# Score products of a two-stage attention and MoE kernel: the keys' low part in half-row products, two heads in turn

## The reference

```python
scores = scale * np.matmul(q, k.transpose(0, 1, 3, 2))
...
scores = scores + bias.transpose(2, 0, 1)[None, :, :, :]
scores = scores - np.max(scores, axis=-1, keepdims=True)
attn = np.exp(scores)
attn = attn / (np.sum(attn, axis=-1, keepdims=True) + 1e-09)
return np.matmul(attn, v)
...
for e in range(E):
    h = np.maximum(x @ w1[e], 0.0)
    ye = h @ w2[e]
    out += P[:, e:e + 1] * ye
```

## Time and profile before

| | us |
|---|---|
| median of 3 runs | 1846.01 (1845.95 to 1847.39) |
| the profiled execution | 1847.22 |
| its span, first to last instruction | 1845.4 |
| TensorE busy in the span | 1829.7 |
| attention, first score product to first expert product | about 61 to 344 |

### The profile page before, as it was taken

One profiled execution on the slowest core, in us unless ns is written; L12 is line 12 of the kernel. 1 busy time (PEld: TensorE's weight loads), 2 busy tenths in 40 slices (PEclk: granted clock), 3 DMA queues, 4 the chain that ended last, 5 costly groups with the idle time before them and its releaser, 6 DMA issues.

```text
span 1845.4 us, 27892 instructions
## 1 busy us (share of the span) xinstructions
PE 1829.7 (99%) x10223; PEld 1592.1 (86%) x10223; DVE 1053.4 (57%) x1784; ACT 824.8 (45%) x1416; POOL 1028.3 (56%) x720
## 2 busy tenths in 40 slices
PE   8999999999999999999999999999999999999999
PEld 4677777788999999999999999999999999999998
DVE  8877777777554555456645554555455445544553
ACT  8777777533433333334333333333333333333331
POOL 0223326577666666666776666666666666666661
PEclk9999999999999999999999999999999999999999
DMA  7763562021112211212121211111121111112110
GB/s 241 226 155 92 128 152 68 23 79 59 69 69 69 69 69 69 69 69 103 69 69 69 69 69 69 69 69 69 69 103 69 69 69 69 69 69 69 69 46 35
DMA packets 44127, 152.47 MB, mean 83 GB/s; under 512 B 9584, under 2 KB 18032, under 8 KB 29680
## 3 DMA queue, kind: packets, MB, share of 16 engines
q1 hardware_dynamic: 44016, 150.99, 25.5%
HBM read 135.63 MB, written 15.34 MB: 82 GB/s over the span
## 4 chain that ended last, share of the span: by engine, by line
PE 94%; DVE 1%; ACT 1%; issue 0%; POOL 0%; ACTq 0%; DVEq 0%; POOLq 0%
PE banks L660 14%; PE banks L661 14%; PE banks L659 14%; PE banks L627 13%; PE banks L631 13%; PE banks L629 13%; PE banks L557 4%; PE banks L518 3%; PE banks L500 3%; PE banks L501 2%; PE banks L571 1%; PE banks L528 0%; DVE h_lo L1167 0%; PE banks L678 0%; ACT probs L786 0%
## 5 line engine op out<-in xcount | busy, mean ns | idle before, releaser
L1279 POOL TENSOR_TENSOR w_lo<-stage,w_hi 128x1024 fp32r<-128x1024 f32 (+1 forms) x288 | 647.5, 2263 | 526.8 <-ACT w_hi L832 525.9
L1161 DVE TENSOR_TENSOR u<-p_copy,banks 128x384 f32<-128x384 f32 x192 | 106.4, 554 | 633.3 <-PE banks L631 633.3
L661 PE MATMUL banks<-w_hi,h_lo 128*128 128x512 f32 x1152 | 450.1, 391 | 0.0
L660 PE MATMUL banks<-w_lo,h_hi 128*128 128x512 f32 x1152 | 449.9, 391 | 0.0
L659 PE MATMUL banks<-w_hi,h_hi 128*128 128x512 f32 x1152 | 449.0, 390 | 0.0
L1167 DVE SCALAR_TENSOR_TENSOR h_lo<-corner,h_hi 128x384 fp32r<-128x384 f32 x384 | 411.1, 1098 | 0.0
L879 ACT ACTIVATE h_hi<-corner 128x384 fp32r<-128x384 f32 x384 | 196.5, 526 | 271.1 <-DVE corner L1161 268.1
L627 PE MATMUL banks<-x_hi,w_hi 128*128 128x384 f32 x896 | 300.6, 336 | 0.6 <-DVE u L1161 0.6
L631 PE MATMUL banks<-x_hi,w_lo 128*128 128x384 f32 x896 | 300.2, 335 | 0.0
L832 ACT ACTIVATE w_hi<-stage 128x1024 fp32r<-128x1024 f32 (+1 forms) x288 | 271.6, 974 | 9.1 <-POOL stage L1273 9.1
L868 ACT ACTIVATE p_copy<-banks 128x384 f32<-128x384 f32 x96 | 47.3, 492 | 491.2 <-PE banks L631 491.2
(11 more groups left out here) (130 smaller groups left out, 2478.3 us busy)
## 6 DMA issues: line engine op xcount, KB each, us to landing
stage<-in_expert_w SPq DMA_DIRECT2D x96, 1024.0 KB, 4.7
raw<-in_qk SPq DMA_DIRECT2D x32, 576.0 KB, 7.1
bias_scratch<-bias_out SPq DMA_DIRECT2D x36, 288.0 KB, 2.6
bias<-bias_scratch SPq DMA_DIRECT2D x16, 288.0 KB, 2.9
v_main<-in_v SPq DMA_DIRECT2D x16, 256.0 KB, 2.7
bias<-bias_scratch SPq DMA_DIRECT2D x16, 256.0 KB, 4.0
out<-total SPq DMA_DIRECT2D x4, 768.0 KB, 4.0
out<-total SPq DMA_DIRECT2D x6, 256.0 KB, 2.0
```

The source lines that it names most:

```text
L660: pe.matmul(dst, h_hi[:, g % 2, f, tokens], lo[:, f], start=False, stop=False)
L661: mm = pe.matmul(dst, h_lo[:, g % 2, f, tokens], hi[:, f], start=False, stop=fp == FPAIRS - 1 and f == 1)
L1161: dve.tensor_tensor(out, other, bank, op).then_inc(combined, 1)
L1279: pool.tensor_tensor(lo, of, hi.bitcast(F32), ALU.subtract).then_inc(w_split, 1)
```

## The change

The operands are laid out anew. The queries of head 0 keep their high part in partitions 0 to 63 and the low part in 64 to 127; head 1 has them the other way round (`high_half`, `low_half`). The product with the high keys stays one of 128 rows, since those keys stand in both halves. The product with the keys' low part now uses only the 64 rows that hold the high part of the queries: rows 0 to 63 for head 0, rows 64 to 127 for head 1. The product of the low queries with the low keys is thereby left out. The order is: column half 0 of head 0 and of head 1, column half 1 of head 0 and of head 1, each with 64 rows into its own bank; then the four products of 128 rows, which add to the banks, with head 0's count after its second.

TensorE now waits for `biased` of both heads before any score product of a step. In the step of 64 queries a `nop` takes the wait. The query differences are two instructions of 64x576 on GpSimd (and for block 0 on VectorE) in place of one of 64x1152, with a wait of GpSimd for its own first one between them; `split_done` counts three per block.

```diff
-                    pe.wait_ge(split_done, 2 * n + 2)
+                    pe.wait_ge(split_done, SPLITS * (n + 1))
...
+                if exists(hp, s - 1):
+                    pe.wait_ge(biased, 2 * at)
+                if rows < P:
+                    pe.nop(nofuse=True)
+                queries_at = slice(qc * P, qc * P + rows)
+                for a in range(2):
+                    cols = slice(HALF * a, HALF * a + HALF)
+                    for h in range(2):
+                        pe.matmul(banks[0:rows, 2 * h + a, 0:HALF], qk_hi[slot][high_half(h), 0, h, queries_at],
+                                  k_lo[slot][high_half(h), h, cols], start=True, stop=False)
                 for h in range(2):
-                    if exists(hp, s - 1):
-                        pe.wait_ge(biased, 2 * at + h - 1)
-                    lhs = qk_hi[slot][:, 0, h, qc * P:qc * P + rows]
                     for a in range(2):
                         cols = slice(HALF * a, HALF * a + HALF)
-                        dst = banks[0:rows, 2 * h + a, 0:HALF]
-                        pe.matmul(dst, lhs, qk_hi[slot][:, 1, h, cols], start=True, stop=False)
-                        mm = pe.matmul(dst, lhs, k_lo[slot][:, h, cols], start=False, stop=True)
+                        mm = pe.matmul(banks[0:rows, 2 * h + a, 0:HALF], qk_hi[slot][:, 0, h, queries_at],
+                                       qk_hi[slot][:, 1, h, cols], start=False, stop=True)
                     mm.then_inc(scores_ready, 1)
...
-                low = slice(D, 2 * D)
-                pool.tensor_tensor(qk_hi[slot][low, 0, :, :], raw[low, slot, 0, :, :],
-                                   qk_hi[slot][low, 0, :, :].bitcast(F32), ALU.subtract).then_inc(split_done, 1)
-
-                pool.wait_ge(split_done, 2 * n + 1)
+                for h in range(2):
+                    low = low_half(h)
+                    pool.tensor_tensor(qk_hi[slot][low, 0, h, :], raw[low, slot, 0, h, :],
+                                       qk_hi[slot][low, 0, h, :].bitcast(F32), ALU.subtract).then_inc(split_done, 1)
+                    pool.wait_ge(split_done, SPLITS * n + h + 1)
```

More of the change, by code:

```diff
@@ L240, in bass_attention_moe @@
         X_PIECES = PAIRS * B
+        SPLITS = 3
         LAST = PAIRS * STEPS
@@ L259, in batch, with high_half, low_half @@
             return hp * B + s // QC, s // QC % 2
+        def high_half(h):
+            return slice(D * h, D * h + D)
+        def low_half(h):
+            return slice(D * (1 - h), D * (1 - h) + D)
         def columns_free(hp, s):
@@ L414, in pairs_of @@
                     if not (last and b >= B - 2):
-                        sp.wait_ge(split_done, 2 * (n + 1))
+                        sp.wait_ge(split_done, SPLITS * (n + 1))
                         load_pair(*((hp, b + 2) if b < B - 2 else (hp + 1, b + 2 - B)))
@@ L837, in round_factor @@
                     act.wait_ge(scores_ready, 2 * (LAST - QC))
-                    act.wait_ge(split_done, 2 * X_PIECES)
+                    act.wait_ge(split_done, SPLITS * X_PIECES)
                     act.wait_ge(scaled, PIECES_0)
@@ L1001, in _ @@
             dve.wait_ge(rounded, 2)
-            dve.tensor_tensor(qk_hi[0][D:2 * D, 0, :, :], raw[D:2 * D, 0, 0, :, :],
-                              qk_hi[0][D:2 * D, 0, :, :].bitcast(F32), ALU.subtract).then_inc(split_done, 1)
+            for h in range(2):
+                dve.tensor_tensor(qk_hi[0][low_half(h), 0, h, :], raw[low_half(h), 0, 0, h, :],
+                                  qk_hi[0][low_half(h), 0, h, :].bitcast(F32), ALU.subtract).then_inc(split_done, 1)
             dve.tensor_tensor(k_lo[0][:, :, :], raw[:, 0, 1, :, :], qk_hi[0][:, 1, :, :].bitcast(F32),
@@ L1252, in split_pair @@
                     pool.wait_ge(rounded, 2 * n + h + 1)
-                low = slice(D, 2 * D)
-                pool.tensor_tensor(qk_hi[slot][low, 0, :, :], raw[low, slot, 0, :, :],
-                                   qk_hi[slot][low, 0, :, :].bitcast(F32), ALU.subtract).then_inc(split_done, 1)
-                pool.wait_ge(split_done, 2 * n + 1)
+                for h in range(2):
+                    low = low_half(h)
+                    pool.tensor_tensor(qk_hi[slot][low, 0, h, :], raw[low, slot, 0, h, :],
+                                       qk_hi[slot][low, 0, h, :].bitcast(F32), ALU.subtract).then_inc(split_done, 1)
+                    pool.wait_ge(split_done, SPLITS * n + h + 1)
                 pool.tensor_tensor(k_lo[slot][:, :, :], raw[:, slot, 1, :, :], qk_hi[slot][:, 1, :, :].bitcast(F32),
                                    ALU.subtract).then_inc(split_done, 1)
-                pool.wait_ge(split_done, 2 * n + 2)
+                pool.wait_ge(split_done, SPLITS * (n + 1))
             def sum_weights(g):
```

## The result

| | before | after |
|---|---|---|
| median, us | 1846.03 (1845.84 to 1847.63, 20 runs) | 1849.05 (1847.57 to 1849.94, 20 runs) |
| span of the profiled execution | 1845.4 | 1847.8 |

The ratio is 1.0014 with a 95% interval of 1.0008 to 1.002: the changed kernel is slower by 0.14%, inside the 0.2% that the prediction called no change and inside its range, but on the other side of the kernel before than its 1845.2. The runs differ in the clock: 15 of the 20 of before stand at 1845.8 to 1846.2 and 5 at 1847.3 to 1847.6, the profiled one among the latter; of the 20 of after 13 stand at 1848.8 and above, with a mean granted clock of 0.998, and the one at 1.000 took 1847.57. The start of attention shows where the lower clock comes from.

A forecast was written before the change was run, and what follows sets the result against it. TensorE, 99% busy, bounds the kernel, then GpSimd's split. Steady blocks -1.7, late block +0.15, last block -0.4, block 0 +0.9, attention's end +0.3 sum to -0.75 us: 1846.01 to 1845.2 us; range 1840.0 to 1854.0, own range 1842.5 to 1848.0.

The forecast's parts named there:

- Half-row products overlap: Attention scores on TensorE: products in different row halves stream and load side by side, four costing two slots, 0.26 us.
- (a): Rival, score products: half products' loads go in turn, 0.11 us each; 0.4 us lost per block, 1853.5 us; chance 0.14.
- (b): Rival, score products: half products don't overlap at all, 0.13 us each; 0.64 us lost per block, 1857 us; chance 0.11.
- TensorE's own saving: Attention scores: 0.055 us less in each of s0, s2, s3, 0.25 in s1, none in s4; 0.41 us per block.
- GpSimd's chain +0.25: GpSimd's split: two query pieces at 1.41 us each plus the wait between add 0.25 us per block.
- The split becomes the bound: Block boundary: GpSimd's split holds back TensorE's next scores, allowing only 0.13 of 0.41 us gained per block.
- The rounding 0.095 earlier: ScalarE's rounding that releases GpSimd: s2's scores 0.305 us earlier, head 0 ready 0.21 later, so it ends 0.095 earlier.
- The wait per block: TensorE's first scores of the next block: a new wait for GpSimd takes some 0.28 us of the 0.41 saved.
- The late blocks: Blocks 13 and 14: the block at 301 us, without slack, loses 0.15 us; together forecast at +0.02.
- Block 0: Attention's start: the second step waits for both heads at half clock, starting near 63.9 us; costs 0.9 us, between 0.3 and 1.2.
- Tail: Attention's end: the last block gains 0.4 us without a split behind it, later head 0 costs 0.3; -0.1 us.
- a new wait of other size: Remaining case: some new wait costs differently than forecast, putting the time between the forecast and (a); chance 0.08.

The follow-up runs named there:

- e2: Changed kernel with GpSimd's split made per head, each head as soon as it is rounded; 1844.94 us, ratio 0.9991 to before.
- e7: Changed kernel with 12, 10 and 6 unread extra products ahead of the scores of block 0's first three steps; 1847.51 us, ratio 1.0007 to before.
- e10: New query layout and three GpSimd instructions, but TensorE's scores in the old order with 128 rows and a wait per head; 1846.89 us, ratio 1.0005 to before.
- e6: e2 with 128 rows for the low keys too, in the new order with the new waits; 1849.98 us (one run).
- e5: e2 with loops over head and column half exchanged, so head 0's two half products come first; 1845.71 us (one run).
- e4: Kernel before the change with only the split made per head (GpSimd's, and VectorE's for block 0); 1847.22 us, ratio 1.0004 to before.
- e1: Changed kernel with block 0 alone in the old order, 128-row products and a wait per head; 1845.97 us, ratio 0.9999 to before.
- e8: Changed kernel with split per head, block 0 in old order, and 12, 5, 3 unread extra products in its first three steps; 1842.99 us, ratio 0.9982.

## Why the prediction was wrong

The steps in the prediction's order.

- **Half-row products overlap: right.** Pairs start together, loads too, 0.13 from pair to pair; (a) and (b) fall. The Trainium skill, TensorE: Matmul & The Clock Gate, section Part 3, gives products in different row groups as concurrent; the trace agrees, here for two groups of 64 rows.
- **TensorE's own saving, 0.41 a block: right in its places, short in what follows.** Mean start-to-start distances over 11 blocks: scores of s0, s2 and s3 shorter by 0.07, 0.065 and 0.08 (forecast 0.055), s1 by 0.20 (0.25), in all 0.41. But s1's transposes, which now come 0.2 us sooner, take 0.08 more: ScalarE's copy of the transposes before them (L810), for whose bank they wait, ends 0.14 us ahead of the first of them in each of the 11 blocks, and s4 takes 0.03 more than before instead of nothing, its gap ahead of the value products having grown from 0.27 to 0.34. Net 0.30. e2 against before, 17.272 - 16.981 = 0.29, confirms the sum.
- **GpSimd's chain +0.25: right.** 30 pieces took 1.41 us each. **The split becomes the bound: right**, shown by e2. **The rounding 0.095 earlier: wrong.** It stands at 10.22 us behind the block's first scores in before and at 10.23 in after: earlier scores and later head 0 cancelled. s2's scores come 0.19 earlier and not 0.305, because s1's scores gain 0.20 and not 0.25 and its transposes take the 0.08 more, and head 0 is ready 0.2 later. So the loop takes 17.215, not 17.14, and a steady block gains 0.057, not 0.13. The wait per block came out at 0.23, forecast 0.28.
- **The late blocks: wrong by 0.37.** Both lost about 0.2. One had no slack, as forecast. In the other, block 14, head 0's rounding came 0.21 us later behind the first scores than before (7.34 against 7.13) and head 1's 0.18 (10.39 against 10.21): here the delay of head 0 is not paid back.
- **Block 0, the failed step.** The second step was forecast at 63.9 and starts at 63.93. I costed that wait once, and it comes twice: the fourth step waits for both heads too, 0.38 us at 71.03 (in before 0.17 for head 0, at 69.15; at full clock 0.23 in e7 and nothing in e10). At full clock, old order (e10) and new (e7), VectorE reads head 0 of the second, third and fourth step at 64.30, 67.11, 69.27 and at 65.21, 68.17, 70.80: later by 0.91, 1.06 and 1.53 us. Block 0 pays 15.12 - 13.68 = 1.44 for the order, where the sum had 0.9. The rest of the 1.68 is the clock: 3.4 us at the lower level cost 14.94 - 13.68 = 1.26 in before, 6.8 us cost 16.62 - 15.12 = 1.50 in after. I had taken before's time at half clock as given. It was not: 13 of the 20 runs of after have 6.8 us of it and none of the 20 of before. And before's median execution has no such time while after's has it, which puts the medians 3.0 apart where the profiled spans are 2.4 apart.
- **Tail: 0.25 more than forecast.** With 128 rows the old order takes 25.58 (e10) and the new one 25.81 (e6), so the order costs 0.23 there, of 0.3 forecast. Half rows then give back 0.07 (e2, 25.74) and not 0.4. At attention's end the chain passes through VectorE, where a TensorE that is early only waits; that this took the 0.33 was not tried by itself.
- **Experts, 0.87: not in the sum, and chance of the profiled execution.** TensorE waits 0.8 us more for VectorE there, and VectorE's `weighed` runs four times its fastest time inside GpSimd's subtraction. What goes with it in all twelve traces is how long one transfer of expert weights takes to land: 4.7 to 5.3 us in the six short ones, 6.0 to 7.5 in the six long ones. When the stretch starts doesn't decide: the six short ones start between 340.21 and 344.16, the six others between 339.64 and 345.69.

The sum in the forecast's terms: 0.78 (block 0) + 0.87 (blocks) + 0.37 + 0.25 + 0.87 (experts) = 3.1, from a forecast span of 1844.6 to 1847.7, measured 1847.8. Of these, the first 0.78 and 0.87 are mis-sized terms, and the last 0.87 is chance.

For the medians block 0 weighs more. Before's median execution is at full clock, so its block 0 is near e10's 13.68, and after's has 6.8 us of half clock: 16.62 - 13.68 = 2.94 us, forecast 0.9. With the blocks (-0.69), the late blocks (+0.39) and the tail (+0.15) that is 2.8 of the 3.0 us between the medians, an estimate from the stretches above, and leaves 0.2 for the experts. So block 0's wait, costed once and without its clock, accounts for 2.0 of the 3.8 us between the forecast 1845.2 and the measured 1849.05. The steady blocks, which gained 0.69 and not 1.56, come second with 0.9. By its time the result lies where the prediction put a new wait of other size (0.08). By its mechanism no rival named it: TensorE's new wait for GpSimd came nearly as forecast, and the wait of block 0 is the one that was mis-sized.

## What to carry to other kernels

Saving time on an engine that is 99% busy is worth the slack of the next loop, no more: write that loop out link by link from one block's first instruction to the next one's, since its period (17.22 here) is the new block, and look for the instruction in it that waits for more than it reads (GpSimd waited for head 1 to split head 0, 0.23 us a block). A wait that is free in the steady state is costed again for every step of the pipeline's first round, with what the clock does around it. And one profiled execution is one draw: a stretch that the change doesn't touch is compared with the spread of the runs before it is explained.

## What the runs showed of the hardware

- Row halves overlap whatever the order of issue: head 0's two half products, then head 1's, span 0.53 us as in turn (e5). In the trace of after a half-row product also starts among 64-row transposes, ahead of two that precede it in the program (270.06 against 270.12 and 270.18).
- A turn from half rows to 128 rows costs 0.09 us of gap and a load of 0.11 that is exposed: 267.33 to 267.79 is 0.46 for 0.26 of streaming. The Trainium skill, TensorEngine Tiling (Array Packing), section Key Properties, says that a change of the mode drains TensorE; here the trace agrees for the turns to and from half rows, s4's entry among them: from the last transpose to the first score product it is 0.20 us now. It does not agree for the same place before, 128\*128 to 128\*64, where it was 0.03 and nothing was lost.
- The `weighed` multiplication on VectorE took 0.31 to 0.89 us where at most 0.1 us of it lay beside GpSimd's subtraction, and 1.04 to 2.54 us inside it, over the twelve traces. The Trainium skill, GPSIMD Engine Reference, section 1. Specifications, names contention for the SBUF interfaces with VectorE instructions that have two SBUF inputs; this one has two, and the trace agrees. VectorE's rounding, with one input, took 1.53 us beside GpSimd's split (e4) and 0.75 without it (e1).
- The changed program ran with a mean granted clock of 0.998 in 13 of 20 executions, 0.999 in 6 and 1.000 in one. Half speed for 6.8 of 1848 us makes 0.998, for 3.4 us 0.999. With the waits of block 0 filled (e7, e8) all 21 executions stood at 1.000.
- A transfer of 1024 KB of expert weights, issued 28.8 us behind the first expert product each time, took 4.7 to 7.5 us from issue to landing over the twelve traces.
